# Gated delta attention on one core: the right side scaled by beta on VectorE inside PSUM, the state's rests on GpSimd, half-width identity parts, and a new order on four engines

## The chip, the cores and the metric

One NeuronCore of a Trainium2 chip runs the whole kernel. The metric is the device time of one execution in microseconds (us). TensorE is written PE, VectorE DVE, ScalarE ACT, GpSimd POOL; SP is the queue that issues the DMAs. "Start to start" is the time from the start of one instruction to the start of the next on the same engine.

## The reference

Three stages run one after the other: a recurrent attention, an MLP with spatial gating, and a token mixer. The change lies in the first.

```python
B, H, S, D = 4, 8, 768, 48
k_n = k / (np.linalg.norm(k, axis=-1, keepdims=True) + 1e-06)
for t in range(S):
    y[:, :, t] = np.einsum('bhd,bhde->bhe', q[:, :, t], state)
    v_old = np.einsum('bhde,bhd->bhe', state, kt)
    state = state + bt[:, :, :, None] * np.einsum('bhd,bhe->bhde', kt, vt - v_old)
# then, on x = y as (B, S, 384):
h = relu(x @ w_in); u, v = halves of h; gated = u * (w_spatial @ norm(v) + b); x = gated @ w_out
theta = x @ w_theta; u = x + w_r @ (x cos theta) + w_i @ (x sin theta); out = u + relu(u @ w_ch)
```

## The kernel before

**Units.** The 768 steps are cut into 12 chunks of 64. A unit is one chunk for two of the four batches: 16 of the 32 states, with two times 64 steps on the 128 partitions. There are 24 units (`NU`); unit u is chunk u//2 of pair u%2, and its state comes from unit u-2. Within a unit the 64 steps are solved at once: a unit triangular matrix N is inverted level by level (`LEVELS` 2, 4, 8, 16, 32), one Newton step corrects it, and the result Z is applied to the right side r = beta * (v - k.state). Numbers are kept as pairs of f16, a high part and a rest.

**The pipeline.** All engines run the same loop over bodies j; in one body the unit x=j is at its first levels, y=j-1 at its last ones, n=j-2 at the solve, the state and the outputs, f=j+1 at its products (q.k, k.k), g=j+2 at the loading of keys and queries. Each engine's order inside a body is written out by hand, and semaphores join them.

**One unit's steps, in order.** POOL `keys`, `key_rests` scale and split the keys; `scaled_masks` makes the mask times beta from rows of beta that SP loads with `beta_load`; PE `products(f,0)` and `(f,1)`, DVE `mask` of each half; POOL `z_even`, `z_odd` put the first Z together; PE `first_t` turns it; then for each level PE `level_w`, two DVE `level_w`, PE `level_t` with ACT `turn`, and PE `level_z` with DVE `level_z`. `level_t` begins with a matmul of 512 columns with the identity that copies T into the bank before the tiles add to it; of what it writes, only the even blocks of the level are read. `level_z` of the last level does the same, and only the odd blocks are read. Then PE `newton`, DVE `newton`, PE `z_rests` with ACT `z_rests`.

**The chain through one PSUM bank pair.** `side_ps` holds one thing after the other: PE `old_keys` (keys times state), DVE `r_firsts` and `r_seconds` (right side, to SBUF `rf`), POOL `r_scaled` (times beta), ACT `r_highs`, DVE `r_rests`, PE `solve`, ACT `u_highs`, DVE `u_rests`, PE `state`, DVE `s_full` (two instructions), PE `old_outputs` and `outputs`, ACT `y_copy`, DVE `y_full`, and then `old_keys` of the next unit. DVE `s_rests` makes the rest of the new state after ACT `s_highs`.

**SP's order in body j.** The key load of unit j+4 waits for `k_read` of unit j+2 (the second instruction of `keys`); then the query load of j+3, two loads of beta rows for j+2, and the v load of j+1, which waits for `r_ready` of unit j-1.

```python
u = j + 4
if live(u):
    need(sp, k_read, u - 1)
    sp.dma_start(kf[u % 2]..., k_dram[u]).then_inc(k_in[u % 2], 16)
...
u = j + 2
if 2 <= u < NU:
    beta_load(u)
```

**POOL's order in body j, before:** `r_scaled(n)`, `a_rests(y)`, `scaled_masks(f)`, `keys(g)`, `z_even(f)`, `key_rests(g)`, `n_rests(x,C)`, `z_odd(f)`, `query_rests(g)`, `x0_rests` in every second body, `n_rests(x,0)`, and in the six bodies 7 to 12 `win_rests`.

Of the kernel before, what the change touches and what calls it, by code (L numbers as in the profile page):

```python
# [17 lines left out]
C = 64  # L18
SIDES = (0, C)
NCH = S // C  # L20
NU = 2 * NCH
# [131 lines left out]
def attention(nc, ctx, whole, q_dram, k_dram, v_dram, beta_dram, rows_dram, win_dram, xT, norm_keys, norm_small, win_raw, win, xs):  # L153
# [99 lines left out]

    def tile(bank, r, h):
        return bank[r:r + C, h * C:h * C + C]
# [13 lines left out]
    def turned(bank):  # L269
        return bank[:].bitcast(F16).rearrange("p (a n c) -> p a n c", a=2, c=P)  # L270

# [68 lines left out]
    def gpsimd(pool):  # L340
# [39 lines left out]
        def n_rests(u, r):  # L380
# [67 lines left out]
        def beta_of(u, n):  # L448
            return cast(beta_up[:, u * H:u * H + H], n, 2)

# [6 lines left out]
        def r_scaled(u):  # L457
            if u == 0:
                pool.wait_ge(beta_ready, 1)
            if carries(u):  # L460
                pool.wait_ge(r_second, n_carried(u + 1))
                r = rf[:]
            else:
                pool.wait_ge(v_in[u % 2], 16 * (u // 2 + 1))
                need(pool, r_high, u)
                need(pool, r_rest, u)
                r = vf[u % 2][:]
            tt(rf[:], r, beta_of(u, D), ALU.mult).then_inc(r_ready, 1)
# [11 lines left out]
        for j in bodies:  # L480
            x, y, n, f, g, o = j, j - 1, j - 2, j + 1, j + 2, j - 5
# [12 lines left out]
            if live(x):  # L494
                n_rests(x, C)
            if live(f):
                z_odd(f)
# [4 lines left out]
            if live(o) and pair_of(o) == 0:  # L502
                x0_rests(o)
# [5 lines left out]
    def scalar(act, values):  # L509
# [107 lines left out]
        for j in bodies:  # L617
            x, y, n, v, f, g = j, j - 1, j - 2, j - 3, j + 1, j + 2
            if live(y):
                turn(y, 1)  # L620
            if live(x):
                n_diags(x, 0)
            if live(v):
                y_copy(v)
            if v == NU - 1:
                values(1)
            if live(x):
                n_diags(x, C)
# [1200 lines left out]
```

## Time and profile before

| | |
|---|---|
| median of 3 runs | 904.62 us (899.27 to 904.77) |
| profiled execution | 896.09 us, span 894.3 us |
| PE busy over the span | 827.6 us (93%) |
| DVE, ACT, POOL busy | 585.5 (65%), 434.3 (49%), 355.4 us (40%) |
| 60 to 360 us: PE, DVE, ACT, POOL busy | 268.76, 262.26, 201.91, 237.86 us of 300 |
| 400 to 894 us: PE busy | 489.48 us of 494 |

The attention lies in the first 400 us, the two dense stages behind it. The profiled execution is 8.5 us under the median of the runs. Busy time of PE counts the modelled tail of each matmul, so start to start is the better measure of it.

### The profile page before, as it was taken

To read this page: it belongs to the slowest core of one execution; us is meant where nothing else is said; L and a number is where in the kernel's file an instruction comes from. 1 tells how busy PE (TensorE), PEld (TensorE's weight loads), DVE (VectorE), ACT (ScalarE), POOL (GpSimd) and SP (SyncE) were. 2 spreads that over 40 slices of the span, in tenths; PEclk is the share of its full clock that TensorE was granted. 3 is DMA by queue.
4 is the path that set the end of the run, shared out by engine and by line. 5 is a ranking of instruction groups with operands and counts; after the bars stand their busy time and mean duration, and the time that the engine had idled before them with its cause. 6 is when DMAs were issued, how large, how long until landed. Compare 5 with 4: busy or idle time off the path is not lost.

```text
span 894.3 us, 30661 instructions
## 1 busy us (share of the span) xinstructions
PE 827.6 (93%) x13224; PEld 755.6 (84%) x13224; DVE 585.5 (65%) x1086; ACT 434.3 (49%) x833; POOL 355.4 (40%) x390
## 2 busy tenths in 40 slices
PE   1889898898889998799999999999999999999998
PEld 1667777777777777679999999999999999999997
DVE  4788898988889888746716526336455834646534
ACT  5676675666567776446224124234344433334221
POOL 5887787968678888314100000000022121121220
PEclk9998998989899999999999999999999999999999
DMA  9624121221122121301000000001410100100101
GB/s 278 207 63 142 47 80 51 68 64 53 57 67 82 59 70 33 118 3 54 1 1 1 1 0 0 0 1 63 168 36 1 54 1 1 53 0 0 54 1 53
DMA packets 26668, 46.56 MB, mean 52 GB/s; under 512 B 2737, under 2 KB 16561, under 8 KB 26545
## 3 DMA queue, kind: packets, MB, share of 16 engines
q1 hardware_dynamic: 26544, 44.74, 15.4%
q8 instruction: 99, 1.62, 0.7%
q14 instruction: 25, 0.20, 0.1%
HBM read 37.85 MB, written 4.72 MB: 48 GB/s over the span
## 4 chain that ended last, share of the span: by engine, by line
PE 69%; DVE 14%; issue 7%; ACT 3%; POOL 3%; SPq 2%; DMA 1%; DVEq 0%; POOLq 0%; ACTq 0%
PE dense_ps L1140 16%; PE dense_ps L1142 16%; PE dense_ps L1141 16%; PE t_ps L915 3%; DVE w_more L724 3%; PE front_ps L880 2%; PE t_ps L911 2%; DVE state_pair L770 2%; PE t_ps L902 2%; PE z_ps L924 2%; DVE rl_pair L749 1%; PE side_ps L1026 1%; DVE z L729 1%; PE extra_ps L1038 1%; DVE w L724 1%
## 5 line engine op out<-in xcount | busy, mean ns | idle before, releaser
L1342 POOL TENSOR_TENSOR vn_f<-vn_f 128x384 f32<-128x384 f32 x24 | 24.5, 1022 | 393.7 <-ACT vn_f L1387 393.7
L1140 PE MATMUL dense_ps<-w_spatial_pair,vn_pair 128*128 128x384 f32 x336 | 112.2, 334 | 0.0
L1141 PE MATMUL dense_ps<-w_spatial_pair,vn_pair 128*128 128x384 f32 x336 | 112.2, 334 | 0.0
L1142 PE MATMUL dense_ps<-w_spatial_pair,vn_pair 128*128 128x384 f32 x336 | 112.2, 334 | 0.0
L724 DVE TENSOR_TENSOR w_more<-t_ps,ident_band_lower 64x256 f16<-64x256 f32 x192 | 80.0, 417 | 8.8 <-PE t_ps L902 5.7
L511 ACT ACTIVATE t<-t_ps 128x512 f16<-128x512 f16 (+1 forms) x144 | 59.9, 416 | 45.8 <-PE t_ps L915 43.1
L1583 DVE TENSOR_TENSOR vn_pair<-vn_f,vn_pair 128x384 fp32r<-128x384 f32 x48 | 31.7, 661 | 58.7 <-ACT vn_pair L1349 58.7
L1141 PEld LDWEIGHTS dense_ps<-w_spatial_pair,vn_pair 128*128 128x128 f32 x336 | 63.1, 188 | 0.0
L1142 PEld LDWEIGHTS dense_ps<-w_spatial_pair,vn_pair 128*128 128x128 f32 x336 | 63.1, 188 | 0.0
L1140 PEld LDWEIGHTS dense_ps<-w_spatial_pair,vn_pair 128*128 128x128 f32 x336 | 63.1, 188 | 0.0
L1519 DVE BATCH_NORM_STATS2 stats<-v_u_f 128x6 f32<-128x512 f32 x24 | 16.7, 694 | 63.2 <-ACT v_u_f L1407 63.1
L902 PE MATMUL t_ps<-t,n_diag 128*128 128x64 f16 x960 | 51.0, 198 | 7.0 <-ACT t L511 4.2
L915 PEld LDWEIGHTS t_ps<-w_more,z 64*64 64x64 f16 x1536 | 33.6, 113 | 26.4 <-issue 26.2
L911 PE MATMUL t_ps<-t,identh 128*128 128x512 f16 x120 | 48.9, 407 | 6.0 <-DVE w_more L724 5.7
L1140 PE MATMUL dense_ps<-w_in_pair,x_pair 128*128 128x512 f32 (+1 forms) x144 | 53.9, 374 | 0.0
L1349 ACT ACTIVATE g_pair<-v_u_f 128x384 fp32r<-128x384 f32 x32 | 16.8, 526 | 74.0 <-DVE v_u_f L1556 74.0
L1142 PE MATMUL dense_ps<-w_in_pair,x_pair 128*128 128x512 f32 (+1 forms) x144 | 52.4, 364 | 0.0
L1141 PE MATMUL dense_ps<-w_in_pair,x_pair 128*128 128x512 f32 (+1 forms) x144 | 52.2, 363 | 0.0
L902 PEld LDWEIGHTS t_ps<-t,n_diag 128*128 128x128 f16 x960 | 40.4, 101 | 12.3 <-ACT t L511 5.5
L1387 ACT ACTIVATE vn_f<-vn_f,quarter 128x384 f32<-128x384 f32 x24 | 14.8, 617 | 70.9 <-DVE vn_f L1577 70.9
L915 PE MATMUL t_ps<-w_more,z 64*64 64x64 f16 x1536 | 45.1, 200 | 0.7 <-issue 0.6
L729 DVE TENSOR_TENSOR z<-z_ps,z 128x256 f16<-128x256 f32 x96 | 40.2, 418 | 3.9 <-PE z_ps L924 2.3
(229 smaller groups left out, 2581.2 us busy)
## 6 DMA issues: line engine op xcount, KB each, us to landing
mask_beta<-in_beta_rows SPq DMA_DIRECT2D x48, 128.0 KB, 3.6
qT_in<-in_q SPq DMA_DIRECT2D x24, 256.0 KB, 4.2
k_in<-in_k SPq DMA_DIRECT2D x24, 192.0 KB, 3.2
v_in<-in_v SPq DMA_DIRECT2D x24, 192.0 KB, 2.3
outT<-g_f SPq DMA_DIRECT2D x6, 576.0 KB, 3.1
w_spatial_f<-in_w_spT SPq DMA_DIRECT2D x3, 768.0 KB, 8.5
w_in_f<-in_k SPq DMA_DIRECT2D x3, 576.0 KB, 8.3
x_f<-in_k SPq DMA_DIRECT2D x3, 576.0 KB, 10.9
```

The source lines that it names most:

```text
L511: return nc.scalar.activation(out, in_, ACT.Copy, scale=scale)
L724: tt(to, odd_even(whole_(ta[u % 2]), l)[r:r + C, :, :, 0, :], keep[r:r + C], ALU.mult).then_inc(w_ready[u % 2], 1)
L729: tt(to, odd_even(whole_(za[u % 2]), l)[:, :, :, 1, :], to, ALU.add).then_inc(z_ready[u % 2], 1)
L770: tt(to[:, :, 1, :], sf[u % 2][:], to[:, :, 0, :], ALU.subtract).then_inc(s_rest, 1)
L902: last = mm(ta[u % 2][:, h * C:h * C + C], nd[u % NS_][:, h, :], t[u % TS][:, h, :], start=True, stop=True)
L911: mm(ta[u % 2][:], identh[:], t[u % TS][:].rearrange("p h c -> p (h c)"), start=True, stop=False, skip_group_check=True)
L915: last = mm(tile(ta[u % 2], r, h), z[u % ZS][r:r + C, h, :], w[l][r:r + C, h, r:r + C], start=False, stop=True, skip_group_check=True)
L1140: mm(out, lhs(LO), rhs(HI), start=first, stop=False)
L1141: mm(out, lhs(HI), rhs(LO), start=False, stop=False)
L1142: return mm(out, lhs(HI), rhs(HI), start=False, stop=last)
L1342: tt(ta[:, r], ta[:, r], xt[:, r], ALU.mult).then_inc(zr_full, 1)
L1583: tt(zs[:, LO, r, n], a[:, r], zs[:, HI, r, n].bitcast(F32), ALU.subtract).then_inc(z_rest, 1)
```

## The change

- `r_scaled` moves from POOL to DVE. For units with a state behind them `r_seconds` writes its result back into `side_ps`, `r_scaled` multiplies it by beta there, and `r_highs` (ACT) and `r_rests` (DVE) read it from there. Units 0 and 1 still use `rf`.
- `s_rests` moves from DVE to POOL.
- The identity matmuls of `level_t` (five a unit) and of the last `level_z` cover the 256 columns that are read.
- POOL takes `scaled_masks` a unit further ahead, for g instead of f, behind `keys(g)`, `key_rests(g)` and `s_rests(v)`.
- The orders inside a body change on PE, DVE, ACT and POOL.

```diff
+    def half_of(a, l, e):
+        return a.rearrange("p (m e s) -> p m e s", e=2, s=LEVELS[l])[:, :, e, :]
+    def right_side(u):
+        return pairs(1) if carries(u) else rf[:]
...
 # POOL, n_rests
-                pool.wait_ge(z_begun, min(u + 2, NU))
+                pool.wait_ge(z_first, min(u + 2, NU))
                 pool.wait_ge(kn_rest, min(u + 3, NU))
+                pool.wait_ge(mb_made, min(u + 3, NU))
+                need(pool, s_rest, n_updates(u - 2))
...
 # POOL, the body
-            if live(n):
-                r_scaled(n)
             if live(y):
                 a_rests(y)
-            if live(f):
-                scaled_masks(f)
             if live(g):
                 keys(g)
+            if live(o) and pair_of(o) == 0:
+                x0_rests(o)
             if live(f):
                 z_even(f)
             if live(g):
                 key_rests(g)
+            if live(v) and updates(v):
+                s_rests(v)
+            if live(g):
+                scaled_masks(g)
+            if live(f):
+                z_odd(f)
             if live(x):
                 n_rests(x, C)
-            if live(f):
-                z_odd(f)
             if live(g):
                 query_rests(g)
...
             if live(x):
                 n_rests(x, 0)
...
 # ACT, r_highs
-            copy(rp[:, :, 0, :], rf[:]).then_inc(r_high, 1)
+            copy(rp[:, :, 0, :], right_side(u)).then_inc(r_high, 1)
...
 # DVE
-            stt(out=rf[:], in0=pairs(1), scalar=-1.0 / UP ** 2, in1=rf[:], op0=ALU.mult, op1=ALU.add).then_inc(r_second, 1)
+            stt(out=pairs(1), in0=pairs(1), scalar=-1.0 / UP ** 2, in1=rf[:], op0=ALU.mult, op1=ALU.add).then_inc(r_second, 1)
+        def r_scaled(u):
...
+            if carries(u):
+                dve.wait_ge(r_second, n_carried(u + 1))
+                r = pairs(1)
...
+            tt(right_side(u), r, cast(beta_up[:, u * H:u * H + H], D, 2), ALU.mult).then_inc(r_ready, 1)
...
-            tt(rp[:, :, 1, :], rf[:], rp[:, :, 0, :], ALU.subtract).then_inc(r_rest, 1)
+            tt(rp[:, :, 1, :], right_side(u), rp[:, :, 0, :], ALU.subtract).then_inc(r_rest, 1)
...
 # PE, level_t, and level_z of the last level
-            mm(ta[u % 2][:], identh[:], t[u % TS][:].rearrange("p h c -> p (h c)"),
+            mm(half_of(ta[u % 2], l, 0), identh[:], half_of(t[u % TS][:].rearrange("p h c -> p (h c)"), l, 0),
...
-                mm(za[u % 2][:], identh[:], z[u % ZS][:].rearrange("p h c -> p (h c)"),
+                mm(half_of(za[u % 2], l, 1), identh[:], half_of(z[u % ZS][:].rearrange("p h c -> p (h c)"), l, 1),
...
 # PE, turn_x
+            need(pe, x_out, u)
```

The rest of the diff is order. In full, for one body after the change:

- PE: `z_rests(n)`, `products(f,0)`, `level_w(y,3)`, `level_t(x,0)`, `solve(n)`, `products(f,1)`, `level_t(y,3)`, `state(n)`, `turn_x(j-3)`, `level_w(x,1)`, `level_z(x,0)`, `level_w(y,4)`, `level_z(y,3)`, `old_outputs(n)`, `outputs(n)`, `level_t(x,1)`, `flip(g)`, `level_z(x,1)`, `level_w(x,2)`, `level_t(y,4)`, `old_keys(y)`, `first_t(f)`, `newton(y)`, `level_z(y,4)`, `level_t(x,2)`, `level_w(f,0)`, `level_z(x,2)`. Before, `level_z(x,1)` stood behind `first_t(f)`, then came `newton(y)`, `level_z(y,4)`, `level_w(f,0)`, `level_t(x,2)`, and `level_z(x,2)` only behind the next body's `level_w(y,3)`; `products(f,1)` stood behind `level_t(y,3)`, and `level_w(x,1)` and `level_z(x,0)` ahead of `state(n)`.
- DVE: `y_full(j-3)`, `level_z(y,1)`, `level_w(y,2)` twice, `r_firsts(n)`, `r_seconds(n)`, `newton(n)`, `r_scaled(n)`, `level_w(x,0)` twice, `r_rests(n)`, `level_z(y,2)`, `mask(f,0)`, `level_w(y,3)` twice, `u_rests(n)`, `mask(f,1)`, `s_full(n)`, `level_w(x,1)` twice, `level_z(x,0)`, `level_w(y,4)`, `level_z(y,3)`, `level_w(y,4)`. Before, `s_rests`, both halves of `level_w(y,3)`, a `level_z` and `mask(f,0)` and then `level_z(y,0)` stood between `r_rests` and `u_rests`.
- ACT: `turn(y,1)`, `x_copy(j-4)`, `turn(n,4)`, `key_T(f)`, `first_t(x)`, `last_z(n)`, `turn(y,2)`, `r_highs(n)`, `z_rests(n)` twice, `turn(x,0)`, `u_highs(n)`, `q_scale(g)`, `query(g)`, `turn(y,3)`, `a_highs(x)`, `s_highs(n)`, `n_diags(f)` twice, `y_copy(n)`.

## Rows read from the trace of the kernel before

**Rows 1.** Timeline, PE: `newton` of units 0, 16, 17, 20 and 22.

```profile
48.79 0.38 PE L934 MATMUL extra_ps<-t,neg_ident 128*128 128x512 f16 x1
...
294.59 0.38 PE L934 MATMUL extra_ps<-t,neg_ident 128*128 128x512 f16 x1
...
308.40 0.38 PE L934 MATMUL extra_ps<-t,neg_ident 128*128 128x512 f16 x1
...
350.93 0.38 PE L934 MATMUL extra_ps<-t,neg_ident 128*128 128x512 f16 x1
...
381.48 0.61 PE L934 MATMUL extra_ps<-t,neg_ident 128*128 128x512 f16 x1
```

**Rows 2.** Timeline, DVE: `r_rests` (L749) in two bodies, `s_rests` (L770) in one.

```profile
221.56 3.74 DVE L749 TENSOR_TENSOR rl_pair<-rf,rl_pair 128x384 f16<-128x384 f32 x1
...
297.20 0.68 DVE L749 TENSOR_TENSOR rl_pair<-rf,rl_pair 128x384 f16<-128x384 f32 x1
297.81 1.62 DVE L770 TENSOR_TENSOR state_pair<-state,state_pair 128x384 f16<-128x384 f32 x1
```

**Rows 3.** Timeline, PE: `solve`, with the idle time ahead of it and what ended it.

```profile
225.45 0.36 PE L979 MATMUL side_ps<-rl_pair,z_rest 128*128 128x48 f16 x8 [2.29 <-DVE rl_pair L749]
```

**Rows 4.** Windows, PE: stretch, its length, PE busy, granted clock, DMA share, GB/s.

```profile
228.00:235.00 7.00, 6.75 (x167) 0.56 0.08 26
```

**Rows 5.** Groups by line, 60 to 360 us: DVE instructions that read `side_ps`.

```profile
L754 DVE TENSOR_TENSOR ul_pair<-side_ps,ul_pair 128x384 f16<-128x384 f32 x20 | 10.8, 541 | 0.0
...
L744 DVE SCALAR_TENSOR_TENSOR rf<-side_ps,rf 128x384 f32<-128x384 f32 x19 | 10.6, 557 | 0.7
```

**Rows 6.** Timeline, PE: a `level_t` in the clean body, and its longest wait.

```profile
292.64 0.38 PE L911 MATMUL t_ps<-t,identh 128*128 128x512 f16 x1
292.95 0.44 PE L915 MATMUL t_ps<-w_more,z 64*64 64x64 f16 x16
...
300.72 0.39 PE L911 MATMUL t_ps<-t,identh 128*128 128x512 f16 x1 [0.44 <-DVE w_more L724]
```

**Rows 7.** Timeline, POOL: one body's instructions, and three of the first bodies.

```profile
26.74 0.83 POOL L436 TENSOR_TENSOR kn<-k_in,rnorm 128x384 f32<-128x384 f32 x1
...
33.41 1.16 POOL L446 TENSOR_TENSOR kq<-qT_in,kq 128x512 f16<-128x512 f32 x1
...
36.47 1.15 POOL L392 TENSOR_TENSOR n_rest<-na,n_diag 64x512 f16<-64x512 f32 x1 [0.24 <-POOL identf L354]
...
215.24 0.68 POOL L417 TENSOR_TENSOR z<-na,ident_band_lower 128x256 f16<-128x256 f32 x1 [2.08 <-DVE na L715]
...
216.68 1.16 POOL L446 TENSOR_TENSOR kq<-qT_in,kq 128x512 f16<-128x512 f32 x1
217.80 1.15 POOL L392 TENSOR_TENSOR n_rest<-na,n_diag 64x512 f16<-64x512 f32 x1
218.91 1.27 POOL L472 TENSOR_TENSOR w_in_pair<-w_in_f,w_in_pair 128x512 fp32r<-128x512 f32 x1
220.15 0.82 POOL L468 TENSOR_TENSOR rf<-rf,beta_up 128x384 f32<-128x384 f32 x1
220.94 1.15 POOL L400 TENSOR_TENSOR a_rest<-na,a_high 128x512 f16<-128x512 f32 x1
222.05 1.26 POOL L455 TENSOR_TENSOR mask_beta<-mask,mask_beta 128x512 f32<-128x512 f32 x1
223.28 0.82 POOL L434 TENSOR_TENSOR kn_pair<-k_in,rnorm 128x384 f16<-128x384 f32 x1
224.07 0.82 POOL L436 TENSOR_TENSOR kn<-k_in,rnorm 128x384 f32<-128x384 f32 x1
...
225.57 0.91 POOL L442 TENSOR_TENSOR kn_pair<-kn,kn_pair 128x384 f16<-128x384 f32 x1
```

**Rows 8.** Timeline, SP: the key load and the two beta loads of one body.

```profile
224.91 0.33 SPq L303 DMA_DIRECT2D k_in<-in_k  x1
...
225.77 1.11 SPq L294 DMA_DIRECT2D mask_beta<-in_beta_rows  x2
```

**Rows 9.** The beta loads' 48 transfers, from issue to landing.

```profile
DMA to landing us min/median/max: 2.8/3.6/7.6
```

More of the change, by code:

```diff
@@ L455, in scaled_masks, with s_rests @@
             tt(mb[u % 2][:, 0], cast(masks[:, 0], H), mb[u % 2][:, 0], ALU.mult).then_inc(mb_made, 1)
[L457 to L468, printed above, removed]
+        def s_rests(u):
+            pool.wait_ge(s_high, n_updates(u + 1))
+            to = st[u % 2][1 - chunk_of(u) % 2]
+            tt(to[:, :, 1, :], sf[u % 2][:], to[:, :, 0, :], ALU.subtract).then_inc(s_rest, 1)
         def win_rests(i):
@@ L650, in scalar @@
             if live(n):
+                r_highs(n)
                 z_rests(n, C)
@@ L794, in vector @@
             x, y, n, v, f = j, j - 1, j - 2, j - 3, j + 1
[L795 to L815 removed]
             if live(v):
                 y_full(v)
+            if live(y):
+                level_z(y, 1)
+            if y == 1:
+                norms(2, (0,))
             if live(y):
@@ L824, in vector @@
                 norms(2, (3,))
-            if live(n) and carries(n):
-                r_firsts(n)
-                r_seconds(n)
-            if live(y):
-                level_z(y, 1)
-            if y == 1:
-                norms(2, (0,))
             if live(n):
+                if carries(n):
+                    r_firsts(n)
+                    r_seconds(n)
                 newton(n)
+                r_scaled(n)
             if live(x):
@@ L842, in vector @@
                 r_rests(n)
-            if live(v) and updates(v):
-                s_rests(v)
+            if live(y):
+                level_z(y, 2)
+            if live(f):
+                mask(f, 0)
             if live(y):
                 level_w(y, 3, C)
-                level_z(y, 2)
                 level_w(y, 3, 0)
@@ L850, in vector @@
                 norms(2, (2,))
+            if live(n):
+                u_rests(n)
             if live(f):
-                mask(f, 0)
+                mask(f, 1)
+            if f == 0:
+                norms(1, range(5))
+                norm_sums(2)
+                norm_sums(3)
             if f == 1:
+                norm_sums(5)
                 norm_sums(4)
@@ L856, in vector @@
                 norm_sums(7)
+            if live(n) and updates(n):
+                s_full(n)
+            if live(x):
+                level_w(x, 1, C)
+                level_w(x, 1, 0)
+                level_z(x, 0)
+            if live(y):
+                level_w(y, 4, 0)
+                level_z(y, 3)
+                level_w(y, 4, C)
     def tensor(pe, values):
@@ L1080, in tensor @@
                 turn_x(v)
+            if live(x):
+                level_w(x, 1)
+                level_z(x, 0)
             if live(y):
@@ L1097, in tensor @@
                 level_t(y, 4)
-            if live(y) and carries(y):
-                old_keys(y)
+                if carries(y):
+                    old_keys(y)
             if live(f):
                 first_t(f)
+            if live(y):
+                newton(y)
+                level_z(y, 4)
+            if y == NU - 1:
+                values(1)
+            if live(x):
+                level_t(x, 2)
+            if live(f):
+                level_w(f, 0)
+            if live(x):
+                level_z(x, 2)
     return Attention(sync, gpsimd, scalar, vector, tensor, na_masked, s_prod, t_ready, z_last, y_out, x_out, x0_rest, win_rest)
```

85 lines of the change are left out of this document (23 added, 62 removed).

## Prediction

> **What bounds the kernel now.** I read the page first: PE is busy 93% of the span, but from 400 us on it is full and the change touches nothing there, so only the first 400 us matter. There I read the timeline for one mark a body, PE's `newton`. From unit 0 to unit 20 it takes 302.1 us, 15.1 a body; the clean body from unit 16 to 17 takes 13.8 [rows 1]. The difference, 1.3 us twenty times, comes in lumps. Their source is seen on DVE: `r_rests`, whose operands both lie in SBUF, takes 0.68 us in one body and 3.74 in another, where it starts while POOL is working through its queue, and `s_rests` takes 1.62 [rows 2]. The reader is to see whom the long one holds up: PE stood idle for 2.29 us ahead of `solve` [rows 3], and after that its granted clock was 0.56 over seven microseconds, nearly all of it at 1.2 GHz, the lower level [rows 4]. In the clean body PE is the bound: its longest wait is 0.44 us [rows 6]. The chain through `side_ps` closes on the same time, since PE's own order fills its gaps.
>
> **What the change takes off DVE.** `s_rests` leaves: 1.62 us a body, from the row; between 0.54 (the nearest instruction of that size, if it ran alone) and 1.62. `r_rests` now has one operand in PSUM like `u_rests`, 0.541 us [rows 5], in place of 0.68 to 3.74 [rows 2]. `r_scaled` comes in: the nearest row is `r_seconds`, 0.557 us, with the same reads from `side_ps`; that the result is written to PSUM is in no row, so I bound it by 0.45 and 0.70 and take 0.56. DVE wins 1.1 us in a clean body and 4.2 in one with a lump, and it hands on to ACT without POOL in between, whose own `r_scaled` took 0.79 [rows 7]. With no DVE instruction left in the loop that has two SBUF operands, I expect the lumps to go: that is 1.3 us a body, if PE is then what sets the pace.
>
> **PE.** Six identity matmuls a body write 256 columns in place of 512. One occupies PE for 0.31 us start to start [rows 6]; half of its columns at 2.4 GHz is 0.107 us, so 0.64 us a body, between 0 (a strided operand that streams at half the rate) and 0.93 (half of 0.31). The Trainium skill speaks against this part: PSUM — Partial Sum Buffer, Specifications, says that a non-contiguous access pattern slows matmuls significantly, and at the first level the halves are runs of two f32. No row shows such a matmul; by that page the saving would be nothing, and PE's loop 13.4. PE's loop would be 13.8 less 0.44 of wait less 0.64, which is 12.7 us, and the new order has to hold the rest of the chain under that. Walked with the rows' durations it does: from `old_keys` through `r_scaled`, `z_rests` on ACT, `solve`, `state`, `s_full`, `outputs` and PE's five steps behind them it closes in about 12.6 (an estimate from those durations, between 12.3 and 13.3; the forecast doesn't use it, the first rival does).
>
> **POOL and SP, where I see the new bound.** `scaled_masks` used to work on the unit f, whose beta rows SP had loaded one body earlier. Now it works on g, and g's rows are loaded in the same body: SP's load of beta for j+2 stands behind the key load of j+4, and that waits for the second instruction of `keys(g)`. So POOL makes `keys(g)`, SP sees it and issues, the rows come, and only then `scaled_masks(g)` can start, with `z_odd(f)` and all else of POOL queued behind it. Before, nobody felt that time. It is a closed cycle, and its length is a sum of rows:
> - From the end of `keys` (224.07 + 0.82 = 224.89 [rows 7]) to the key load's issue 0.02, to the pair of beta loads 0.88, to the second of them half of 1.11 more [rows 8]; landing 3.6 after issue [rows 9]; together 5.0, and 0.1 to wake: 5.1.
> - `scaled_masks`, 222.05 to 223.28: 1.23.
> - `z_odd`, two instructions, 215.24 to 216.68: 1.44.
> - `n_rests(x,C)`, 1.12, with a wait on POOL's own results ahead of it and behind it; such a wait cost 0.24 once, I take 0.26 for both: 1.38.
> - `query_rests` 1.12, `n_rests(x,0)` 1.11, `a_rests` 1.11, `keys` 1.61 [rows 7].
>
> The sum is 14.1 us a body. `z_even`, `key_rests`, `s_rests` (the nearest is `key_rests`, 0.91) and `x0_rests` stand between `keys` and `scaled_masks` and lie inside the 5.1: the moved `s_rests` costs nothing as long as POOL waits there, and 0.91 if it doesn't. In six bodies `win_rests` adds 1.24 outside of it. PE meets the cycle in `first_t(f)`, which needs `z_odd(f)`. POOL's lead over PE there is at most some 4 us, and the first bodies use it up.
>
> **The start.** `keys` of unit 2 ended at 27.57. With 5.1, 1.23 and 1.44 behind it, `z_odd(1)` ends at 35.4, where it was done by 33.4. One more cycle of 14.1, with 1.9 for the constants made in that body (3.06 less 1.12, [rows 7]), puts `z_odd(2)` at 51.4 and `newton` of unit 0 at 51.8, against 48.8: a loss of 3.0, between 1 and 5, as the queue is also full of first loads then (7.6 is the longest landing [rows 9]).
>
> **The sum.** `newton` of unit 20 comes at 51.8 + 20 x 14.1 + 6 x 1.24 = 341.2, against 350.9: 9.7 won. From body 22 there is no beta to load, and the two bodies that took 30.6 [rows 1] should take about 28: 2.5 more. The dense stages follow as they are. So the profiled execution would take 896.1 - 12.2 = 884, and the median, which is 8.5 above that execution, 904.6 - 12.2 = 892.
>
> **Rivals.** *The beta rows come earlier, and POOL is no bound.* If they land in 2.8 us, the shortest row, the cycle is 13.3 and the end 16 us before my forecast, 876; if POOL keeps ahead altogether, PE's 12.7 rules, 28 less and 3 for the start: 862. The middle is 868. For it: half the loads land sooner than 3.6. Against it: they are behind the key and query loads in one queue, and they were in the same place when they took 3.6. The Trainium skill, DMA: Bandwidth & Descriptors, Anatomy of one DMA, gives 2.0 us and the bytes at 436 GB/s, for the path through GpSimd; for 128 KB that is 2.3, and by it the cycle would be 12.8 and this rival the forecast. This trace doesn't agree: 2.8 at the least.
>
> *Slower: PE's wait brings its clock down in every body.* Where POOL paces, PE waits some 1.4 us at `first_t(f)`. A wait of 0.44 did nothing, one of 2.29 was followed by seven microseconds at 0.56; 1.4 lies between. If each body pays 7 x 0.44 = 3.1 us, it takes 12.7 + 3.1 = 15.8, `newton` of unit 20 comes at 368, and the end 14.5 later than now: 919. It decides from 15.1 us a body on. Against it: after a fall PE is late, has nothing to wait for, and POOL catches up, so falls should come in every second body at most, and the mean stays near 14.1 to 14.3.
>
> *Nothing gained.* Falls in part of the bodies and beta loads whose issue is stretched give 14.7: then the end is where it was, 904.
>
> *The lumps stay.* POOL has no free moment in the old body, and if it is PSUM or the f16 operand that must wait, `r_rests` still takes 3.7 now and then. POOL's pace would hide a part of it; the time would be about 900. I count it with the third.
>
> **How the numbers follow.** The forecast, POOL's cycle of 13.8 to 14.5 us, has 0.52; the early rows 0.17; nothing gained 0.19; slower by the clock 0.12. My own case alone spans 884 to 900 (0.3 us a body either way is 6 us, the start 2). The range is 868 to 908: it leaves out half of the early rows, and the clock rival. This kernel's runs tell about 1% (9 us) from no change. Of my case three quarters lie below 895.6, with all of the early rows: faster 0.56. The rest of mine and nearly all of the third: same 0.30. Slower 0.14.
>
> **What the profile after should show.** POOL waiting for the DMA of `mask_beta` ahead of `scaled_masks` in some 20 bodies, 2 to 3 us each; PE waiting for POOL's `z` ahead of `first_t`; `r_rests` at 0.54 and no instruction of DVE over 1 us in the loop; `scaled_masks` at 1.26 throughout; the identity matmuls 0.1 us shorter start to start; `newton` marks 14.1 apart, 15.3 in the six bodies with `win_rests`. If the marks are under 13.2 apart and POOL doesn't wait for a DMA, the cycle is not where I put it. If they are over 15 with the clock under 0.9, it is the clock. If `r_rests` still shows 3.7, the reason for the lumps was wrong.

## The result, and the profile after

The changed kernel took 907.21 us (median of 20 runs, 902.18 to 914.62), the kernel before 900.33 us on the same chip (884.22 to 906.99). The recorded ratio is 1.0162, 95% interval 1.0125 to 1.02; it sets all twenty executions of the changed kernel against the seven fastest of the kernel before, whose others count as slow because they lie over 1.5% above its fastest one, while the medians alone give 1.008 and the means of all executions 1.009. So the changed kernel is slower by 0.8 to 1.6%, where I had forecast 12 us less. The profiled execution took 904.33 us, its span is 902.6.

The first lines of the page say that no engine works longer: PE 828.3 us (827.6 before), DVE 558.9 (585.5), POOL 344.1 (355.4).

```profile
span 902.6 us, 30681 instructions
PE 828.3 (92%) x13224; PEld 766.7 (85%) x13224; DVE 558.9 (62%) x1088; ACT 439.0 (49%) x833; POOL 344.1 (38%) x388
```

The same mark as in [rows 1], PE's `newton`, now of units 0, 2, 16, 17, 20 and 22:

```profile
54.50 0.39 PE L936 MATMUL extra_ps<-t,neg_ident 128*128 128x512 f16 x1
...
90.45 0.39 PE L936 MATMUL extra_ps<-t,neg_ident 128*128 128x512 f16 x1
...
303.59 0.39 PE L936 MATMUL extra_ps<-t,neg_ident 128*128 128x512 f16 x1
318.26 0.39 PE L936 MATMUL extra_ps<-t,neg_ident 128*128 128x512 f16 x1
...
359.20 0.39 PE L936 MATMUL extra_ps<-t,neg_ident 128*128 128x512 f16 x1
...
389.61 0.61 PE L936 MATMUL extra_ps<-t,neg_ident 128*128 128x512 f16 x1
```

Before, unit 0 was at 48.79, unit 20 at 350.93 and unit 22 at 381.48 [rows 1], and unit 2 at 79.81 in the same timeline. So 5.7 us are lost by unit 0 and 10.6 by unit 2, and from there to unit 22 it is 299.2 us against 301.7: the loop gained 2.5. The table of waits between 60 and 360 us (engine and line, what it waited for, us in total, times, longest) names what took the place of the lumps:

```profile
POOL mask_beta L461 <- DMA mask_beta<-in_beta_rows: 62.1, 18, 8.0
...
DVE na L711 <- POOL a_rest L409: 15.0, 15, 2.0
PEld t_ps L894 <- POOL z L428: 10.3, 12, 2.1
```

POOL waits for beta's rows in 18 bodies, 3.5 us each, and behind it DVE and PE wait for POOL. One body of POOL's timeline, with SP's:

```profile
202.33 0.83 POOL L445 TENSOR_TENSOR kn<-k_in,rnorm 128x384 f32<-128x384 f32 x1
...
208.57 1.26 POOL L461 TENSOR_TENSOR mask_beta<-mask,mask_beta 128x512 f32<-128x512 f32 x1 [2.73 <-DMA mask_beta<-in_beta_rows]
...
211.59 1.15 POOL L401 TENSOR_TENSOR n_rest_more<-na,n_diag 64x512 f16<-64x512 f32 x1 [0.31 <-issue]
```
```profile
203.19 0.33 SPq L310 DMA_DIRECT2D k_in<-in_k  x1
203.57 0.43 SPq L314 DMA_DIRECT2D qT_in<-in_q  x1
204.04 1.11 SPq L301 DMA_DIRECT2D mask_beta<-in_beta_rows  x2
```

From the end of `keys` (203.16) to `scaled_masks` are 5.41 us. The mean over the loop is 5.5. One body has more, and its reason is a load that I hadn't counted:

```profile
76.38 0.43 SPq L344 DMA_DIRECT2D w_in_f<-in_w_in  x1
...
77.86 1.17 SPq L301 DMA_DIRECT2D mask_beta<-in_beta_rows  x2
```
```profile
86.75 1.27 POOL L461 TENSOR_TENSOR mask_beta<-mask,mask_beta 128x512 f32<-128x512 f32 x1 [7.96 <-DMA mask_beta<-in_beta_rows]
```

The 1.5 MB of `w_in`, a weight of the next stage, stand ahead of beta's rows in SP's queue once, and from the end of `keys` (76.66) to `scaled_masks` it is 10.1 us there. DVE did what was forecast: `r_scaled` in PSUM takes 0.56, `r_rests` 0.54 from unit 2 on (0.56 for the last two), where it had been 0.56 to 0.68 in most bodies and 2.17, 3.74, 3.74 and 3.75 in four of them [rows 2].

```profile
214.78 0.56 DVE L753 TENSOR_TENSOR side_ps<-side_ps,beta_up 128x384 f32<-128x384 f32 x1
216.17 0.54 DVE L758 TENSOR_TENSOR rl_pair<-side_ps,rl_pair 128x384 f16<-128x384 f32 x1
```

But units 0 and 1 still take their right side from SBUF, and their `r_scaled` is on DVE now: 1.17 us for unit 0 and, below, 2.12 for unit 1. The next fence has windows of the changed kernel (stretch, length, busy times of PE, PEld, DVE, ACT and POOL, granted clock, DMA share, GB/s): PE's clock was near the lower level from 60 to 70 us, where the kernel before had 1.00, and 0.72 in the whole stretch from `newton` of unit 0 to that of unit 2. The third fence is the same stretch in the kernel before.

```profile
73.86 2.12 DVE L753 TENSOR_TENSOR rf<-v_in,beta_up 128x384 f32<-128x384 f32 x1
```
```profile
60.00:70.00 10.00, 10.00 (x230) 8.58 (x226) 7.56 (x18) 5.52 (x12) 5.25 (x7) 0.53 0.27 84
54.50:90.45 35.95, 31.38 (x790) 27.09 (x786) 28.54 (x54) 20.05 (x41) 22.72 (x24) 0.72 0.30 98
```
```profile
48.79:79.81 31.02, 26.92 (x791) 22.00 (x788) 26.80 (x51) 19.70 (x42) 23.27 (x25) 0.89 0.35 113
```

So 4.9 us are lost between the two marks, and 4.5 of them are PE's own work, which took 31.4 us in place of 26.9 at the lower clock; what PE waited for is nearly the same (4.6 and 3.8 us). Two rows stand ahead of the fall: PE had waited 2.30 us for POOL's `z`, which is the cycle of beta's rows, and then 0.96 for a `level_w` of DVE, which stood behind a step of the key norms that itself had waited 4.01 us for ACT (that these two alone brought the clock down isn't shown):

```profile
54.13 0.44 PE L894 MATMUL t_ps<-ident_band_lower,z 64*64 64x64 f16 x16 [2.30 <-POOL z L428]
```
```profile
55.58 0.24 DVE L688 TENSOR_SCALAR x_f<-x_f 128x144 f32<-128x144 f32 x1 [4.01 <-ACT x_f L517]
```

The identity matmul over half the columns, and the next one's start, 0.22 us later (0.31 in [rows 6]; 0.20 to 0.22 in most of the bodies):

```profile
209.87 0.29 PE L913 MATMUL t_ps<-t,identh 128*128 128x256 f16 x1
210.09 0.44 PE L917 MATMUL t_ps<-w_more,z 64*64 64x64 f16 x16
```

### The profile page after: what moved, and what is told of

Read it like the earlier page. It is cut to its first block, busy times and chain, and to the rows that moved or that the text cites. A ratio compares the mean times of both kernels' runs of the same rounds, so it can differ in the third digit from the quotient of the medians.

```text
span 902.6 us, 30681 instructions
## 1 busy us (share of the span) xinstructions
PE 828.3 (92%) x13224; PEld 766.7 (85%) x13224; DVE 558.9 (62%) x1088; ACT 439.0 (49%) x833; POOL 344.1 (38%) x388
## 4 chain that ended last, share of the span: by engine, by line
PE 55%; issue 2%; DVE 2%; ACT 2%; POOL 1%; POOLq 0%; ACTq 0%; DVEq 0%
PE dense_ps L1143 16%; PE dense_ps L1144 16%; PE dense_ps L1145 16%; PE t_ps L917 1%; PE dense_ps L1661 1%; PE t_ps L904 1%; PE dense_ps L1660 1%; POOL vn_f L1347 1%; PE z_ps L926 1%; ACT w_spatial_pair L1352 0%; PE side_ps L1028 0%; ACT vn_f L1390 0%; PE extra_ps L1041 0%; PE side_ps L986 0%; PE front_ps L882 0%
## 5 line engine op out<-in xcount | busy, mean ns | idle before, releaser
L461 POOL TENSOR_TENSOR mask_beta<-mask,mask_beta 128x512 f32<-128x512 f32 x24 | 30.7, 1279 | 78.3 <-DMA mask_beta<-in_beta_rows 72.7
L904 PE MATMUL t_ps<-t,n_diag 128*128 128x64 f16 x960 | 53.0, 202 | 1.3 <-ACT t L509 0.7
L711 DVE TENSOR_TENSOR na<-front_ps,mask_beta 128x512 f32<-128x512 f32 x48 | 32.9, 685 | 25.1 <-POOL a_rest L409 17.6
L882 PE MATMUL front_ps<-kq 64*64 64x128 f16 x768 | 33.4, 238 | 16.3 <-POOL kq L455 7.7
```

Source lines behind the costliest of these rows:

```text
L461: tt(mb[u % 2][:, 0], cast(masks[:, 0], H), mb[u % 2][:, 0], ALU.mult).then_inc(mb_made, 1)
L711: tt(na[u % 2][:, HP * i:HP * i + HP], front[:].rearrange("p (n a c) -> p n a c", n=HP, a=2), mb[u % 2][:, :, HP * i:HP * i + HP].rearrang ...
L882: last = mm(front[r:r + C, n * P:n * P + P], kq[u % KQ][d, b, n, 0, r:r + C], kq[u % KQ][d, o, n, :, r:r + C], start=e == 0, stop=e == 2)
L904: last = mm(ta[u % 2][:, h * C:h * C + C], nd[u % NS_][:, h, :], t[u % TS][:, h, :], start=True, stop=True)
```

## The experiments

The runs were made in four groups, each on a chip of its own; a ratio is to the kernel before on the same chip, whose median was 904.91, 900.97, 899.25 and 904.97 us. My theory after the result: two costs, the cycle of beta's rows and the start, stand against the gain from the lumps. The rivals: the new order itself is slow, the half products or DVE's writes to PSUM cost, the clock falls.

### The cycle of beta's rows: e1, e2, e4, e6

e1_beta_first: the changed kernel, in SP's pass the beta load ahead of the key load.

```diff
+            u = j + 2
+            if 2 <= u < NU:
+                beta_load(u)
             u = j + 4
             if live(u):
                 need(sp, k_read, u - 1)
```

> The changed kernel with one edit: in SP's body the two beta loads of unit j+2 stand ahead of the key load of j+4, so they no longer wait for the second instruction of keys. My theory (POOL waits for the beta rows in a closed cycle with SP, 5.5 us from the end of keys to scaled_masks, 14.9 us a body) expects that wait to be gone in nearly all bodies, marks of newton about 13.0 to 13.5 apart, and 870 to 880 against some 900 for the kernel before. First rival: the new order itself, or PE's waits with the clock at its lower level, is what costs; then the wait on POOL goes to another place, the marks stay over 14.3, and the time stays at 900 or more. Second rival: only the start was lost (some 10 us), then 895.

897.76 us, ratio 0.9931 (0.9889 to 0.9974). The gain is there, but the wait isn't gone (57.7 us in 19 bodies). The time lies between the theory (870 to 880) and the first rival (900 or more), nearest to the second rival's 895. In one of the bodies the beta load stood behind the values' load of the pass before, which waits for `r_scaled`:

```profile
266.92 0.33 SPq L341 DMA_DIRECT2D v_in<-in_v  x1
267.29 1.11 SPq L301 DMA_DIRECT2D mask_beta<-in_beta_rows  x2
```
```profile
272.35 1.28 POOL L461 TENSOR_TENSOR mask_beta<-mask,mask_beta 128x512 f32<-128x512 f32 x1 [4.14 <-DMA mask_beta<-in_beta_rows]
```

Between units 3 and 19 a body takes 14.7 us, where the changed kernel takes 15.1; 13.0 to 13.5 was not reached.

e2_masks_for_f: the changed kernel, POOL's `scaled_masks` back to the unit f.

```diff
             if live(y):
                 a_rests(y)
+            if live(f):
+                scaled_masks(f)
             if live(g):
                 keys(g)
...
-            if live(g):
-                scaled_masks(g)
```

(And `n_rests` waits for one `mb_made` less.)

> The changed kernel with scaled_masks for unit f again, behind a_rests(y), as in the kernel before; all else of the change stays. My theory: the beta rows were loaded a body earlier, no wait, the time falls to 870 to 885; it may lie a little over the one with the earlier loads, since mask(f,0) now waits for a scaled_masks of 1.26 us that stands just ahead of it. Rival (order or clock): no gain, 900 or more.

898.57 us, ratio 0.9963 (0.9927 to 0.9998), neither 870 to 885 nor 900 or more. No wait for the rows, POOL waits for DVE's `na` instead (62.6 us in 20 bodies), a body at 14.5.

e4_masks_g_on_before: the reverse, that move alone on the kernel before.

```diff
-            if live(f):
-                scaled_masks(f)
...
                 key_rests(g)
+            if live(g):
+                scaled_masks(g)
```

(And `n_rests` waits for `mb_made` of u + 3.)

> The kernel before with the suspected cost alone: scaled_masks works on g, behind key_rests(g), and nothing else is changed. My theory: POOL's cycle is keys, beta rows, masks, rests, z, then all the rest of its body with r_scaled in it, near 15.5 to 16.5 us a body against 15.1 now, and 5 more at the load of w_in; so 10 to 30 us slower than the kernel before. Rival: the position of scaled_masks is free, and the time stays within 3 us.

936.74 us, ratio 1.039 (1.0323 to 1.0456): 3.9% from one moved instruction, a little more than the 10 to 30 us expected.

```profile
POOL mask_beta L456 <- DMA mask_beta<-in_beta_rows: 71.3, 18, 5.8
```

e6_beta_before_values: the changed kernel, the rows loaded one pass earlier.

```diff
-            u = j + 2
+            u = j + 3
             if 2 <= u < NU:
                 beta_load(u)
```

(It stands where it stood, between the queries' and the values' loads.)

> The changed kernel with the load of beta's rows moved in SP's queue alone: the rows of the unit three ahead stand in front of the values' load of the same pass, one pass earlier, so that they wait for the masks of the body before only, and no longer for r_scaled, nor stand behind the window's 1.5 MB load. If the cycle from the masks over the load to GpSimd's scaled masks set the main loop, GpSimd's wait for the DMA (91 us before the 24 scaled masks in the changed kernel) falls under 8 us and the time to that of the best order so far or below: 894 to 899 us, a body at 14.0 to 14.4. If the loop is closed at about 14.8 by something else (the chain of levels over TensorE, ACT and DVE), the wait moves to another engine and the time stays within 3 us of the changed kernel's 907. In both cases the 8 to 10 us lost by unit 2 stay.

895.14 us, ratio 0.9944 (0.9905 to 0.9982), with POOL's order untouched. Its waits for a DMA are gone; it waits for DVE's `na` instead (67.6 us in 21 bodies), as in e2, and this costs less. A body takes 14.5, and the start is as late as before (`newton` of unit 2 at 91.73). So the cycle is a cost of the change and is taken away by one number in SP's queue. That e2, from POOL's side, gives the same body of 14.5 says that the cycle was the same thing in both.

### The right side in PSUM alone, and the start: e5, e7

e5_psum_part_on_before: the kernel before, `r_scaled` on DVE in PSUM, `r_rests` from there, `s_rests` on POOL, all orders else as they were.

```diff
-            stt(out=rf[:], in0=pairs(1), scalar=-1.0 / UP ** 2, in1=rf[:], op0=ALU.mult, op1=ALU.add).then_inc(r_second, 1)
+            stt(out=pairs(1), in0=pairs(1), scalar=-1.0 / UP ** 2, in1=rf[:], op0=ALU.mult, op1=ALU.add).then_inc(r_second, 1)
...
                 newton(n)
+                r_scaled(n)
```

> The kernel before with the first part of the change alone: r_scaled on DVE inside PSUM, r_rests reading PSUM, s_rests on POOL in the place that r_scaled had; old order, whole identities. My theory: the long r_rests (3.7 us, three times, and one of 2.2) go, and with them PE's spells at the lower clock; 15.1 us a body becomes about 14, so 15 to 30 us faster. Rival: what DVE saves is not on the path (PE paces the clean body at 13.8), and only the three lumps of 4.7 us go: 10 to 15 us. Second rival: the lumps move to another instruction, no gain.

888.44 us, ratio 0.9874 (0.9809 to 0.9939): 11 us by the ratio, 16 by the medians, where the theory had 15 to 30 and the first rival 10 to 15. The lumps are gone, a body takes 14.4 (15.1 before): they were worth 0.7 us a body, not the 1.3 that I had given them. But unit 2 comes at 86.59, 6.8 us later than before. DVE's timeline shows why; the third line is the same `r_scaled` for unit 1:

```profile
50.26 3.58 DVE L688 TENSOR_SCALAR x_f<-x_f 128x144 f32<-128x144 f32 x1 [0.40 <-ACT x_f L515]
54.37 1.06 DVE L753 TENSOR_TENSOR rf<-v_in,beta_up 128x384 f32<-128x384 f32 x1
...
69.86 2.50 DVE L753 TENSOR_TENSOR rf<-v_in,beta_up 128x384 f32<-128x384 f32 x1
```

These are DVE instructions whose inputs all lie in SBUF, and POOL is at work. e6 shows the pattern at its barest, the same instruction with POOL idle (unit 0) and with POOL working through a queue (unit 1), and POOL's lines beside the second:

```profile
58.35 0.55 DVE L753 TENSOR_TENSOR rf<-v_in,beta_up 128x384 f32<-128x384 f32 x1
...
74.71 3.04 DVE L753 TENSOR_TENSOR rf<-v_in,beta_up 128x384 f32<-128x384 f32 x1
```
```profile
74.34 0.91 POOL L451 TENSOR_TENSOR kn_pair<-kn,kn_pair 128x384 f16<-128x384 f32 x1
75.21 0.91 POOL L466 TENSOR_TENSOR state_pair<-state,state_pair 128x384 f16<-128x384 f32 x1
76.08 1.25 POOL L461 TENSOR_TENSOR mask_beta<-mask,mask_beta 128x512 f32<-128x512 f32 x1
```

It starts at 74.71 and ends at 77.75, 0.42 behind the end of POOL's last one (77.33): it waited for three POOL instructions, not for one. The Trainium skill, SBUF — State Buffer, SBUF: two separate sides, says that a DVE instruction with two SBUF inputs and a GpSimd instruction exclude each other for a whole instruction, whoever starts first. These rows agree on the exclusion; that DVE is passed over by several POOL instructions that follow each other without a gap is more than that.

e7_psum_part_start_on_pool: e5, with the `r_scaled` of units 0 and 1 on POOL as before.

```diff
+            if live(j - 2) and not carries(j - 2):
+                r_scaled_first(j - 2)        # POOL
...
+                if carries(n):
+                    r_scaled(n)              # DVE
```

> As e5_psum_part_on_before (the kernel before with the right side scaled on DVE inside PSUM, its rest read from there, and the state's rest on GpSimd), but the right sides of units 0 and 1, which come from SBUF, are scaled on GpSimd as before. If the 6.8 us that e5 lost by unit 2 come from DVE instructions with both operands in SBUF (r_scaled of units 0 and 1 at 1.06 and 2.50 us, TensorE idle 2.08 behind the second, the clock at half), the mark of newton(2) falls from 86.6 to 80 to 83 us and the time to 882 to 886 us. If the loss comes from another place of the start (the norms' instructions, 3.58 us at 50 us), newton(2) stays at 85 to 87 us and the time at 888.

883.57 us, ratio 0.9772 (0.9711 to 0.9832). The time met the first reading, the mark didn't: unit 2 at 85.59. `r_scaled` of the first two units was at most a small part. The norms' step took 3.19 us (at 51.85) and `r_rests` of unit 1, whose input is still in SBUF, 2.54 (at 72.19), and PE stood idle 2.75 and 1.85 us behind them. In the kernel before the norms' step had started at 49.82, while POOL was at work, and got through between two of its instructions in 0.53. That was luck: in e3 (below), which has the kernel before's orders and only shorter products, the same step took 3.33 us and `newton` of unit 2 came at 85.87.

```profile
52.34 3.33 DVE L696 TENSOR_SCALAR x_f<-x_f 128x144 f32<-128x144 f32 x1 [0.40 <-ACT x_f L523]
```

So the 10.6 us are counted against an execution of the kernel before that had a good start.

### The half products: e3, e8

e3_half_on_before: the kernel before with the half products alone. e8_psum_half_start_on_pool: e7 with them.

```diff
-            mm(ta[u % 2][:], identh[:], t[u % TS][:].rearrange("p h c -> p (h c)"),
+            mm(half_of(ta[u % 2], l, 0), identh[:], half_of(t[u % TS][:].rearrange("p h c -> p (h c)"), l, 0),
```

> The kernel before with one part of the change alone: each of the six identity products of a unit writes 256 columns (the half that has no product of its own) in place of 512. The changed kernel's trace has such a product at 0.20 to 0.21 us from start to start, against 0.31 before. If TensorE's own work sets the body (my prediction's claim once the lumps on DVE are gone), some 0.6 us of each of 22 bodies come off: 14 us, 891 us. If the lumps on DVE and the chain through the other engines set it (what the runs so far say), the saved time turns into idle time of TensorE: 0 to 4 us off, 901 to 905 us. Slower by more than 3 us is expected by neither.

> As e7_psum_part_start_on_pool, with the identity products over half the columns. With the lumps on DVE gone, TensorE is nearer to setting the body, so the half products should be worth more than on the kernel before: if TensorE's stream sets the body, 0.6 us in each of 22 bodies, 10 to 14 us under e7; if the chain of levels through ACT and DVE does, 2 to 6 us under e7 (a level's chain gets 0.1 us shorter for each identity product that stands ahead of its level's own). No gain at all would say that GpSimd's or DVE's stream sets it.

e3: 901.15 us, ratio 0.9968 (0.9927 to 1.001); e8: 885.85, ratio 0.9783 (0.9709 to 0.9858) against e7's 0.9772. No gain that these runs can tell, though each product is 0.1 us shorter. The 14 us of the first reading lie outside what the intervals allow (7 us for e3, 8 for e8 against e7); the marks between units 3 and 19 are 0.26 us a body closer in e8 than in e7 (14.19 and 14.45), which would be 5 us and is not seen in the times. So the sum of PE's busy time alone doesn't set the body.

### A start without the collisions: e9 to e12

For units 0 and 1 ACT copies the values into PSUM and DVE scales them there; the five steps of the norms' last group go behind the first mask, where POOL mostly waits for one (the first of them still took 1.91 us in e9 and 0.80 in e10).

```diff
+        def v_up(u):                         # ACT, units 0 and 1
+            act.wait_ge(v_in[u % 2], 16 * (u // 2 + 1))
+            need(act, y_out, u)
+            copy(pairs(1), vf[u % 2][:]).then_inc(r_second, 1)
...
                 mask(f, 0)                   # DVE
+            if y == 1:
+                norms(2, (0, 1, 2))
+            if y == 2:
+                norms(2, (3, 4))
```

e9 is e6 with it, e10 is e8 with it (and with no `r_scaled` on POOL), e11 is e10 with full products, e12 is the changed kernel with it.

> The kernel e6_beta_before_values (changed kernel, beta's rows ahead of the values' load), and a start without DVE instructions that read two operands in SBUF while GpSimd is at work: for units 0 and 1 ACT copies the values into PSUM, where DVE scales them, and the norms' five steps of the third group stand behind the first mask of bodies 2 and 3, where GpSimd waits for a mask. In e6 such instructions took 2.61 (norms, at 54.3 us), 1.89 (norms, 72.2) and 3.04 us (r_scaled of unit 1, 74.7), and TensorE stood idle 3.52 and 2.42 us behind them. If they are the start's loss, newton(2) comes at 84 to 87 us in place of 91.7 and the time falls to 888 to 891 us. If the new order's own chain sets the start, newton(2) stays at 89 us or later and the time at 893 to 896.

> The same start on the kernel before's order: right side scaled and its rest taken in PSUM for all units (units 0 and 1 copied there by ACT), state's rest on GpSimd, half identity products, norms' steps at the end of bodies 2 and 3. In e7 the norms' step took 3.19 us at 51.9 and the rest of unit 1, still from SBUF, 2.54 at 72.2; TensorE stood idle 2.75 and 1.85 behind them. If that is the loss of the start, newton(2) comes at 80 to 82 us as in the kernel before (79.8) in place of 86, and the time at 878 to 881 us, ratio 0.970 to 0.975. If not, it stays at 884 and newton(2) at 85 or later. Against e9, which has the same parts and only another order on each engine and scaled_masks for the unit two ahead: if the new order costs nothing, the two are within 4 us; what e6 and e8 showed (14.5 against 14.2 us a body) says e9 is 8 to 12 us slower.

> As e10_psum_half_start_norms but with the full identity products. If half products are worth only what e7 and e8 showed (nothing that could be measured in the times, 0.2 us a body in the marks), it comes out 0 to 4 us above e10: 880 to 884 us. If TensorE's stream sets the body now that the start's loss is gone, 8 us or more above e10.

> The changed kernel with the start of e9 alone, beta's rows loaded where the change has them. If the start's loss and the cycle of beta's rows are two separate costs that add, newton(2) falls from 90.5 to 84 to 87 us and the time to 900 to 903 us, about 10 us above e9. If the cycle takes the gain back (GpSimd's scaled masks of units 3 to 5 wait for rows that the loads at 76 us delay), the time stays at 905 to 908 us with newton(5) near 132.9 as in the changed kernel.

| | us | ratio (95%) | `newton` of unit 2 |
|---|---|---|---|
| e9 | 889.14 | 0.9871 (0.9819 to 0.9923) | 81.68 |
| e10 | 884.01 | 0.984 (0.9774 to 0.9905) | 79.02 |
| e11 | 886.62 | 0.981 (0.9741 to 0.988) | 80.72 |
| e12 | 904.45 | 1.0055 (1.0019 to 1.0092) | 84.73 |

Of the times, e9's and e11's are as the first reading had them, e10's is 3 us and e12's 1.5 us above it. The marks of e9 and of e10:

```profile
81.68 0.39 PE L945 MATMUL extra_ps<-t,neg_ident 128*128 128x512 f16 x1
```
```profile
79.02 0.38 PE L950 MATMUL extra_ps<-t,neg_ident 128*128 128x512 f16 x1
```

The mark falls wherever the start is the only difference: by 10.0 us from e6 to e9, by 7.1 from e8 to e10, by 5.7 from the changed kernel to e12. Each mark is of one execution; e14 below, which has e9's start, has it at 83.55, 1.9 later. From unit 0 to unit 2 e12 takes 30.8 us, like the kernel before (31.0), where the changed kernel takes 35.9, and PE is busy 26.1 of them at a clock of 0.94:

```profile
53.93:84.73 30.80, 26.13 (x788) 22.37 (x786) 25.16 (x53) 21.11 (x44) 20.81 (x24) 0.94 0.35 114
```

So what the start lost behind unit 0 lies in what this edit takes away. That is two things at once: the collisions of DVE with POOL, and the wait for ACT that the norms' first step handed on to the steps of DVE behind it (4.01 us in the changed kernel, 2.76 in e6). No run tells them apart. The 5.7 us lost by unit 0 it leaves nearly as they are (`newton` of unit 0 at 53.93 against 54.50 and 48.79); the runs without the cycle have that mark at 53.05 (e6), 50.88 (e9) and 52.94 (e14), so some 1 to 3 of the 5.7 are the cycle's (e6 against the changed kernel, e9 and e14 against e12) and the rest is open.

Of the time less is kept: 0.9944 to 0.9871 for e9 and 1.0162 to 1.0055 for e12, which is 7 and 10 us (4 us for e12 by the means of all executions, 1.009 to 1.005); for e10 nothing that can be told from e8 (the intervals overlap). With the changed kernel, e6, e12 and e9 there are four corners: the cycle costs 2.2% (changed kernel to e6) or 1.8% (e12 to e9), the start 1.1% or 0.7%; with the 1.009 of all executions in place of 1.0162, the first of each pair is 1.6% and 0.4%. The cycle's cost stands clear of the noise in both pairs, the start's cost in time doesn't: the intervals of e6 and e9 overlap by 0.2%, and the 1.1% hangs on which executions of the kernel before are counted. Without both, the change would be 1.3% faster than the kernel before. The new order shows no gain: e9 and e10 hold the same parts in the new and in the old order, 889.14 and 884.01 us on one chip, their intervals overlapping. The best version is the PSUM part in the old order, with or without the rest (e7, e8, e10, e11: 0.977 to 0.984).

### What closes the body now: e13, e14

With lumps and cycle gone a body takes 14.2 to 14.7 us in either order, and PE hardly waits for anybody. From 100 to 300 us e10's PE is idle 21.4 us in 34 places for "issue", which is time in which it waited for nothing that the profile shows, and 0.5 for other engines. Two of these gaps, both in the middle of a loop of like matmuls, so that no semaphore can be meant:

```profile
217.77 0.41 PE L931 MATMUL t_ps<-w_more,z 64*64 64x64 f16 x14
218.78 0.22 PE L931 MATMUL t_ps<-w_more,z 64*64 64x64 f16 x2 [0.61 <-issue]
...
221.87 0.18 PE L985 MATMUL side_ps<-state_pair,kq 64*64 64x48 f16 x1
222.67 0.21 PE L985 MATMUL side_ps<-state_pair,kq 64*64 64x48 f16 x1 [0.61 <-issue]
```

Between them lie 126 matmuls. All of e10's gaps over 0.45 us from 115 us to 254 are 125 to 127 matmuls apart, or near to a multiple of that (250 to 253, 377, 503 and 504). The DMA queues of the same 200 us (packets, MB, share) hold a queue of kind instruction, 16 KB a packet: 49 packets, for some 14 bodies of about 440 matmuls, are one for some 125 matmuls, every four us.

```profile
q8 instruction: 49, 0.80, 1.7%
```

Only the rate is the same: packets of this queue lie between 216.0 and 216.5 us, 220.0 and 220.5, 223.5 and 224.0, and the gaps end at 218.78 and 222.67. That the packets make the gaps isn't shown.

e13_fewer_loads_old_order (e10) and e14_fewer_loads_new_order (e9) cut the loads that these packets could queue behind:

```diff
-                sp.dma_start(kf[u % 2][:].rearrange("p h d -> p (h d)"), k_dram[u])
+                rows = slice(0, P if u < 2 else 1)
+                sp.dma_start(kf[u % 2][rows].rearrange("p h d -> p (h d)"), k_dram[u][rows])
```

> As e10_psum_half_start_norms, but from unit 2 on the loads of keys and values fetch one partition of 128 (the kernel computes with the keys and values of units 0 and 1 from there on): 384 of the 896 KB of a body no longer move, the instructions are the same. If the gaps of TensorE's instruction stream (idle for issue, 20 us or more between 100 and 300 us, some 1.4 us a body) come from packets of instructions that queue behind the loads, they shrink by a third or more and the time by 8 to 12 us against e10: 872 to 876 us. If they belong to the stream itself, a packet of 16 KB each 121 to 125 matmuls whatever else moves, the time stays within 4 us of e10's 884 and the sum of the gaps within a fifth.

> As e9_start_and_beta_on_after (the changed order with both costs taken away), with the same cut of the keys' and values' loads. The same two readings: 877 to 881 us if the gaps are queueing behind loads, within 4 us of e9's 889 if not. TensorE's busy time per body stays at 13.2 us, against 12.7 in the old order, in both: then the new order's cost is in the matmuls' own durations (weight loads less well hidden), not in its waits.

e13: 877.23 us, ratio 0.9702 (0.963 to 0.9774); e14: 884.09, 0.9771 (0.9705 to 0.9838): 1.4% under e10 and 1.0% under e9, with intervals that touch or overlap theirs, so that both times lie between their two readings. The gaps shrink by less than the third that queueing asked for: from 21.4 to 19.3 us in e13, within the fifth of the other reading, and from 16.5 to 12.6 in e14. So most of them don't come from queueing behind the keys' and values' loads; for the quarter that goes in e14 it is open. What the 1% is stays open too. PE's granted clock was 1.00 in e13 against 0.98 in e10, but the clock alone isn't it: e7 and e11 had 1.00 over the same 200 us, and bodies of 14.5 and 14.7. PE is busy 13.2 to 13.3 us a body in the new order and 12.6 to 12.8 in the old, in both pairs; the mean durations of most groups differ by a few ns only, and I can't say where the half microsecond comes from.

## Why the prediction was wrong

The loop's main mechanism was the forecast one and the sign was not. That 907 lies inside the range of 868 to 908 is no credit: against the kernel before, the change costs 7 us by the medians where 12 were to be won. By the sum, `newton` of unit 20 should have come at 341.2; it came at 359.2. The 18.0 us between them fall on three places: 2.7 by unit 0, 7.8 from unit 0 to unit 2 (36.0 for two bodies, not 28.2), 7.5 from there to unit 20 (18 bodies at 14.93, not 14.51 with the `win_rests`). Two more went behind unit 20 (30.4 us for two bodies, not 28).

- **The start, the step that failed most.** I gave it 3.0 us, 1 to 5, as a loss of POOL's by unit 0, and let the loop's pace begin there. It was 5.7 by unit 0 and 10.6 by unit 2. The first part has in it the mechanism that I had, larger: the first rows of beta held `scaled_masks` from 27.60, the end of `keys`, to 35.23, which is 7.6 us and not 5.1 (the runs without the cycle give back 1 to 3 us of this part; the rest is open). For the second part, 4.9 us, the sum has no term. I had walked the start along the beta cycle alone, though I had named the rule that breaks it: "With no DVE instruction left in the loop that has two SBUF operands". The diff says that units 0 and 1 still use SBUF, and they are where `r_scaled` came to DVE: 1.17 and 2.12 us, and 1.43 for `r_rests` of unit 1, where some 0.5 would do. The norms' first step wasn't held by POOL in the changed kernel (0.24), but it waited 4.01 us for ACT, with the levels' steps behind it; in e5, e6 and e7 it was held (3.58, 2.61, 3.19). On PE it shows as the clock: at 0.72 from unit 0 to unit 2, where it was 0.89, the same work took 4.5 us longer, of the 4.9. I had the clock as a rival for the loop and at nothing for the start. e9 and e12 take collisions and wait away together, and unit 2 comes 10.0 and 5.7 us earlier.
- **The cycle's length, a term mis-sized.** 5.1 us from `keys` to `scaled_masks` were 5.5 in the mean, and the rest of POOL's cycle took 9.2 where the sum has 9.0. At unit 20 that is 7.5 us, 0.42 a body. The load of 1.5 MB in SP's queue, which I had not looked for, lengthened one cycle by 4.6, in the body that ends with unit 2; there it lies under the start's other losses. By e2, e4, e6 and the pair of e12 and e9 the cycle is the right mechanism: moving `scaled_masks` costs 1.6 to 2.2%. e1 shows it in part only, since its loads came to wait for something else.
- **What the cycle stood against.** I gave the lumps 1.3 us a body, and e5 wins 0.7 without them. And I took what was left without the cycle as PE's 12.7 us a body. With lumps and cycle gone it is 14.2 to 14.7: PE is busy 12.6 to 13.3 of it, so the sum of PE's work was near, but 1.2 (e9) to 1.6 us a body (e10) are gaps in its instruction stream. They are in the kernel before too (8.7 us between 100 and 300) and I had read over them. So the rival at 862 had no ground, and the range reached too far down for it.
- **Right:** `r_scaled` in PSUM (0.56 taken, 0.56 measured), `r_rests` (0.54 and 0.54, no lump left in the loop), `scaled_masks` (1.26 throughout), POOL's wait for beta's rows in 18 to 20 bodies (3.5 us each, where I had 2 to 3), PE's wait for POOL at `first_t`, the moved `s_rests` at no cost (0.91 inside the wait).
- **The half products:** 0.107 us each was right as a duration (0.31 to 0.20 or 0.22); as a gain it was nothing that the times show, and 0.2 to 0.3 us a body at most by the marks (e7 and e8, e11 and e10), not 0.64. I had put them in PE's loop as if PE's work set it. Of the Trainium skill's rule on non-contiguous access in PSUM (PSUM — Partial Sum Buffer, Specifications) the rows show nothing: products written in runs of two f32 and longer had the next start 0.20 to 0.22 us later, which is 0.31 less the 0.107 of the columns left out. The measurement decides here.
- **The rivals.** The clock did not fall in every body (0.96 from 100 to 300 us, 0.94 before), but it did in the start, where no rival had it. "Nothing gained", at 14.7 a body, describes the loop well. It missed by 7 us all the same (the profiled executions differ by 8.2), as no case of mine had a start of 10 us in it.

## What to carry to other kernels

Walk the first bodies by themselves, and in them the branches of the code that only they take: what a change removes from the loop it can bring into the start. One execution of the kernel before can be lucky there, so read the start in a second one. When work on a buffer is moved ahead, look at the queue that fills the buffer: everything that stands ahead of the load there, once in the whole run too, is part of the new cycle; here one number in SP's loop (`j + 3` for `j + 2`) was worth some 2%. And before an engine's work is called the bound, subtract its busy time from the clean body and find out what the rest is: a shorter instruction gains little while gaps of another kind close the loop.

## What the runs showed of the hardware

- A DVE instruction with both inputs in SBUF that starts while POOL has a full queue can be passed over by several of POOL's instructions: 3.04 us over three of them in e6, 0.55 us with POOL idle. One with a single input in SBUF and scalars was held too (the norms' step: 3.58 us in e5, 3.19 in e7, but 0.24 in the changed kernel, where it started between two instructions of POOL).
- PE's instruction stream has gaps, mostly of 0.5 to 1.9 us, near multiples of 125 matmuls apart (e10), with 16 KB packets of an instruction queue at the same rate. In a loop of small matmuls (about 440 in 14.5 us) this was 1.2 us a body in e9 and 1.6 in e10.
- DVE can read and write the same place in PSUM at the price of a write to SBUF: 0.56 us for 128x384 f32, against 0.557 for `r_seconds` before.
